# Pooled attention outputs spread and added by TensorE in the prologue, with a new order for prologue and block 0

## What is computed

```python
# q, k, v: (4, 8, 576, 64)
q_d, k_d, v_d = (x.reshape(B, H, 144, 4, D).mean(axis=3) for x in (q, k, v))
out_up = np.repeat(softmax_attention(q_d, k_d, v_d), 4, axis=2)
mask = np.abs(pos[:, None] - pos[None, :]) < 4
out_local = softmax(where(mask, scale * q @ k.T, -1e9)) @ v
x = (out_up + out_local).transpose(0, 2, 1, 3).reshape(2304, 512)
h = x @ w_in                      # (2304, 2048)
out = (h * tanh(softplus(h))) @ w_out
```

## Time and profile before

| what | us |
|---|---|
| median of 3 runs | 493.91 |
| lowest and highest of them | 490.74, 494.74 |
| the profiled execution | 491.38 |
| its span, first to last instruction | 489.6 |
| mean granted TensorE clock | 0.996 |

### The profile page before, as it was taken

The page is one execution under the profiler, slowest core; times in us unless marked ns, Lnnn a source line. Parts: engine busy times, 40 slices in busy tenths (PEclk is TensorE's granted clock), DMA queues, the critical chain, the costliest instruction groups (busy, mean ns, idle before and its releaser), DMA issues.

```text
span 489.6 us, 10818 instructions
## 1 busy us (share of the span) xinstructions
PE 476.7 (97%) x4364; PEld 427.5 (87%) x4364; DVE 238.4 (49%) x495; ACT 201.5 (41%) x434; POOL 112.9 (23%) x188
## 2 busy tenths in 40 slices
PE   7789999999999999999999999999999999999997
PEld 6678988889898989889898989898998998999995
DVE  4867897553663553544535525435355343222220
ACT  3688285644642533524514525234345151201111
POOL 4899524213303303123112022022021010000000
PEclk8999999999999999999999999999999999999999
DMA  7993093222232130430310301101211000100001
GB/s 244 323 385 114 11 313 111 80 88 97 77 109 59 52 109 23 153 109 1 109 39 20 121 14 45 58 1 57 76 47 57 23 0 2 66 0 1 0 1 64
DMA packets 23729, 39.89 MB, mean 81 GB/s; under 512 B 2688, under 2 KB 12160, under 8 KB 23680
## 3 DMA queue, kind: packets, MB, share of 16 engines
q1 hardware_dynamic: 23680, 39.21, 25.0%
HBM read 34.48 MB, written 4.72 MB: 80 GB/s over the span
## 4 chain that ended last, share of the span: by engine, by line
PE 88%; DMA 3%; POOL 3%; issue 3%; SPq 2%; DVE 1%; ACT 0%; POOLq 0%; DVEq 0%
PE banks L716 39%; PE banks L731 39%; PE banks L666 2%; PE banks L647 2%; PE banks L586 2%; PE banks L619 2%; DMA v_in<-in_v 1%; PE banks L601 1%; PE banks L629 1%; DMA k_t<-in_k 1%; DMA w_out_raw<-in_w_out 1%; POOL prob L474 1%; SPq L334 1%; POOL q_halves L445 1%; POOL v_pool L468 0%
## 5 line engine op out<-in xcount | busy, mean ns | idle before, releaser
L946 DVE CAST g_high<-banks 128x384 fp32r<-128x384 f32 x96 | 53.4, 556 | 163.1 <-PE banks L731 123.5
L716 PE MATMUL banks<-x_high,w_in_high 128*128 128x384 f32 x384 | 130.8, 341 | 1.2 <-DVE g_low L948 1.2
L716 PE MATMUL banks<-x_high,w_in_low 128*128 128x384 f32 x384 | 129.4, 337 | 0.0
L716 PE MATMUL banks<-x_low,w_in_high 128*128 128x384 f32 x384 | 128.8, 336 | 0.0
L1139 ACT ACTIVATE banks<-banks 128x384 f32<-128x384 f32 x96 | 45.4, 476 | 196.1 <-PE banks L716 195.9
L731 PE MATMUL banks<-w_out_high,g_high 128*128 128x512 f32 x288 | 115.1, 400 | 0.0
L731 PE MATMUL banks<-w_out_high,g_low 128*128 128x512 f32 x288 | 113.4, 394 | 0.0
L731 PE MATMUL banks<-w_out_low,g_high 128*128 128x512 f32 x288 | 113.1, 393 | 0.0
L474 POOL TENSOR_TENSOR prob<-prob,small 128x432 f32<-128x432 f32 x24 | 22.3, 928 | 255.3 <-DVE small L907 255.3
L716 PEld LDWEIGHTS banks<-x_high,w_in_high 128*128 128x128 f32 x384 | 72.1, 188 | 5.6 <-DVE g_low L948 2.4
L716 PEld LDWEIGHTS banks<-x_low,w_in_high 128*128 128x128 f32 x384 | 72.1, 188 | 2.8
(11 more groups left out here) (72 smaller groups left out, 478.2 us busy)
## 6 DMA issues: line engine op xcount, KB each, us to landing
v_win<-in_v_win SPq DMA_DIRECT2D x24, 256.0 KB, 3.5
v_in<-in_v SPq DMA_DIRECT2D x32, 168.0 KB, 4.2
k_t<-in_k SPq DMA_DIRECT2D x16, 290.0 KB, 4.7
q_t<-in_q SPq DMA_DIRECT2D x24, 192.0 KB, 3.7
out<-stage SPq DMA_DIRECT2D x17, 256.0 KB, 2.3
k_win<-in_k_win SPq DMA_DIRECT2D x20, 216.0 KB, 3.7
w_out_raw<-in_w_out SPq DMA_DIRECT2D x16, 256.0 KB, 5.3
w_in_raw<-in_w_in SPq DMA_DIRECT2D x16, 256.0 KB, 8.4
```

Source lines behind the costliest of these rows:

```text
L716: last = nc.tensor.matmul(hidden[:, g % HB, 0:TB], w, x[:, k, cols], start=(k == 0 and i == 0), stop=(k == KT - 1 and i == 2))
L946: nc.vector.tensor_copy(g_high[:, g % GB], x).then_inc(g_rounded, 1)
```

## The change

1. For units 0 to 3 `pooled_outputs`, `upsample` and `combine` are replaced by `first_outputs`. PE reads each probability four times (a broadcast of step 0), so one matmul has 192 columns in place of 96, and writes straight to the token columns of the band's output. A pass of `spread_outputs` has 6 matmuls; a second pass with the two banks swapped adds the other half of the keys. PE waits for its own first pass before the second, and for the second before the window's matmuls, which now add to what stands there. The factor 1/4 moves into `copy_pooled`.
2. `round_x(n)` of these units waits for `out_ready` in place of `combined`.
3. All five lists of the prologue and of block 0 are in a new order; from block 1 on nothing moves but one pair of maxima.
4. `busy_for_turns` and `busy_for_outputs` calls are partly replaced by `busy_for_products`, zeros that wait for the last softmax of the prologue.

```diff
+                def spread_outputs(n, swap):
                     s = work(n)
+                    for step in range(CHUNKS):
+                        for part in range(2):
+                            i = (0, 1, 2)[step] if part == 0 else (1, 2, 0)[step]
+                            h, r = (2 * i + part) // CHUNKS, 1 - part if swap else part
+                            rows, some = slice(WK * part, WK * part + CK), slice(GQ // 2 * r, GQ // 2 * (r + 1))
+                            last = nc.tensor.matmul(
+                                x_out(n)[D * h:D * (h + 1), r].rearrange("p (t g o) -> p t g o", t=GT, o=POOL),
+                                v_pool[rows, 0, n, D * i:D * (i + 1)],
+                                s["prob_pool_t"][rows, i, :, some].rearrange("p t (g o) -> p t g o", o=1).broadcast_to(
+                                    [CK, GT, GQ // 2, POOL]),
+                                start=not swap and step != 1, stop=False)
+                    last.then_inc(out_spread, 1)
+                def first_outputs(n):
                     pe.wait_ge(prob_copied, 2 * n + 2)
                     if 1 <= n < AHEAD - 1:
                         pe.wait_ge(x_split, n)
+                    pe.wait_ge(v_pooled, n + 1)
+                    spread_outputs(n, False)
+                    pe.wait_ge(out_spread, 2 * n + 1)
+                    spread_outputs(n, True)
+                    pe.wait_ge(out_spread, 2 * n + 2)
+                    window_outputs(n)
...
-                                        start=True, stop=True)
+                                        start=n >= AHEAD, stop=n >= AHEAD or tp == TP - 1 and c == 1)
...
                 def combine(n):
-                    dve.wait_ge(up_ready, n + 1)
-                    nc.vector.scalar_tensor_tensor(up[:, n % 2], out_pool(n)[:, 1], 1.0 / POOL, up[:, n % 2], ALU.mult,
-                                                   ALU.add).then_inc(up_added, 1)
+                    dve.wait_ge(up_ready, n - AHEAD + 1)
+                    nc.vector.tensor_tensor(up[:, n % 2], out_pool(n)[:, 1], up[:, n % 2], ALU.add).then_inc(up_added, 1)
...
                 def round_x(n):
-                    act.wait_ge(combined, n + 1)
+                    if n < AHEAD:
+                        act.wait_ge(out_ready, n + 1)
+                    else:
+                        act.wait_ge(combined, n - AHEAD + 1)
```

More of the change, by code:

```diff
@@ L363, in _ @@
                 load_q(0)
+                load_q(2)
+                load_const()
                 load_v(0)
-                load_const()
                 load_k(0)
+                load_v_win(0)
                 load_w_out(0)
-                load_q(2)
                 load_q(1)
-                load_v_win(0)
                 load_k(1)
+                load_q(4)
                 load_w_in(0)
-                load_q(4)
                 load_v(1)
                 load_k(2)
-                load_w_in(2)
                 load_k(3)
                 load_w_in(1)
+                load_w_out(1)
+                load_w_in(2)
                 load_q(3)
-                load_w_out(1)
+                load_v(2)
                 load_v(3)
-                load_k_win(4)
[L383 to L394, removed]
+                load_v_win(1)
+                load_v_win(3)
+                load_w_in(5)
+                load_w_in(3)
+                load_v_win(2)
+                load_v_win(4)
+                load_w_in(4)
+                load_v(4)
+                load_masks()
+                load_k(4)
+                load_w_out(2)
+                load_k_win(4)
                 for f in range(6, FT):
@@ L514, in _ @@
                 low_in(4)
+                pool_v(4)
                 low_in(5)
@@ L696, in busy_for_outputs, with busy_for_products @@
                     keep_busy(BUSY, out_bank(n)[:, 0, 0:P])
+                def busy_for_products():
+                    pe.wait_ge(shifted, AHEAD)
+                    pe.wait_ge(exp_pool, AHEAD)
+                    keep_busy(BUSY, hidden[:, 0, 0:P])
                 def first_product(j, f, tiles=range(KT)):
@@ L743, in _ @@
                 band_scores(1)
-                pooled_scores(1)
                 keep_busy(BUSY)
                 keep_busy(BUSY)
+                pooled_scores(1)
+                turn_pooled(0)
                 turn_band(0)
                 band_scores(2)
+                first_outputs(0)
                 pooled_scores(2)
-                keep_busy(BUSY)
-                turn_pooled(0)
-                keep_busy(BUSY)
-                turn_band(1)
-                outputs(0)
                 turn_pooled(1)
                 band_scores(3)
+                turn_band(1)
+                busy_for_outputs(1)
                 pooled_scores(3)
+                first_outputs(1)
+                busy_for_turns(2)
                 turn_band(2)
                 turn_pooled(2)
-                busy_for_outputs(1)
-                outputs(1)
-                busy_for_turns(3)
-                busy_for_turns(3)
-                band_scores(4)
-                busy_for_turns(3)
+                busy_for_products()
+                busy_for_products()
+                first_outputs(2)
                 turn_pooled(3)
-                outputs(2)
                 turn_band(3)
-                pooled_scores(4)
-                outputs(3)
+                busy_for_products()
+                busy_for_products()
+                first_outputs(3)
                 first_product(0, 0, range(KT - 1))
```

206 lines of the change are left out of this document (101 added, 105 removed).

## The result

| what | before | changed |
|---|---|---|
| median of 19 executions, us | 493.06 | 496.02 |
| the profiled execution, us | 491.38 | 499.04 |
| its span, us | 489.6 | 497.2 |
| mean granted TensorE clock in it | 0.996 | 0.990 |
| start of the first product in it, us | 32.6 | 40.0 |

The ratio is 1.0054, with an interval of 1.0029 to 1.0078: about 2.6 us slower, inside the forecast's range (494.0, 489.5 to 498.5) and in its class of "within 1%". One of the 19 executions of the changed kernel, at 565.5 us, was slow for a reason of its own (without it the median is 495.5), and the ratio here and all ratios and medians of the experiments leave out such executions. The two profiled executions stand 7.7 us apart, the medians 2.4 to 3.0, so part of what they show is not the change but which execution was profiled; the experiments sort that out.

A forecast was written before the change was run, and what follows sets the result against it. The prologue was taken as a dependence chain through five strict queues, then PE's own time. Profiled 491.4 + 2.0 - 0.8 = 492.6; on the mean, 492.7 + 1.2, rounded to 494.0 us, range 489.5 to 498.5.

The forecast's parts named there:

- +2.0 for the product's start: Prologue: the first product was to start at 34.5 us, 2.0 us later than in the kernel before.
- -0.8: Block 0: PE's 0.5 us at a pooled transpose and 0.3 us of late weight loads were to go.
- wrong if the first product starts ... after 36.5: Sign of a failed forecast: first product before 32.5 or after 36.5 us, or new block 0 PE waits over 0.5.
- the walk: Prologue: durations followed through the changed engine lists, plus 0.6 us for gaps, put the first product at 34.5 us.
- SP: ... nothing: SP's load list: the new wait for `out_ready` was to cost nothing, with 2 MB still in the queue.
- The spread: Units 0 to 3 on PE: 2.5 us a unit against 1.0 before, with 1.55 us saved behind it.
- rival D: Passes on PE: by the page's latency formula, 0.35 us shorter each, -2.1 us in all, 491.9; chance 0.10.
- In the old kernel unit 3's summing lay under the first 18 matmuls, and the new passes stand ahead of them.: Start of the first product: why the spread, even for x at +1.5 and -1.55 us, was not even there.
- Rival A: Prologue: clock at half rate, 1.6 us a unit for units 0, 2 and 3, 4.8 in all, 498.8; chance 0.15.
- Unit 4's keys: SP's loads: these keys were to come at about 30 us, ahead of two low parts of x, hidden.
- Rival B: SP's loads: unit 4's keys land after 33 us; landing at 35 gives +2, 496; chance 0.05.
- rival C: Prologue: ACT and DVE queues overlap better, outputs end at 31.0 us, -1.5 and -0.8, 490.4; chance 0.20.

The follow-up runs named there:

- e12: The change unaltered, measured again on the chip of the last four runs: 495.95 us, ratio 1.0021 to before.
- e1: The changed kernel with one load moved, unit 4's queries going behind unit 3's in SP's list: 492.98 us, ratio 0.9969 to before.
- e7: The changed kernel with unit 4's queries moved behind unit 3's and unit 3 alone summed the old way: 490.91 us, ratio 0.9949 to before.
- e11: e7 without one of the two `busy_for_products` (zeros only) ahead of unit 3's outputs: 491.10 us, ratio 0.9939 to before.
- e3: The changed kernel's spread on PE with all five lists in the order of before: 495.52 us, ratio 1.0032 to before.
- e4: The changed kernel's new lists with the old summing on ACT and DVE: 495.13 us, ratio 1.0030 to before.
- e10: The changed kernel with before's whole load list, the other four lists new: 497.60 us, ratio 1.0074 to before.
- e5: The kernel before with one load moved, unit 4's queries going behind unit 3's: 493.28 us, ratio 0.9966 to before.
- e6: Old summing on ACT and DVE in the new lists, with unit 4's queries moved behind unit 3's: 494.09 us, ratio 0.9992 to before.
- e2: The changed kernel with six more multiplications of zeros on PE ahead of unit 2's band scores: 495.38 us, ratio 1.0012 to before.
- e9: e1 without the zeros PE multiplies after unit 1's band transposes (six calls): 496.43 us, ratio 1.0039 to before.

## Why the prediction was right, and where it was not

- **The time.** 494.0 was forecast, 495.5 to 496.0 measured; sign, class and range are right. The sum behind it is not, so this was in part luck. The sum was for the profiled execution, 492.6, and that came at 499.04. Its two terms were +2.0 for the product's start and -0.8 behind it; measured were +7.4 (40.0 against 32.6; +5.2 in e12) and +0.2. By the forecast's own sign ("wrong if the first product starts ... after 36.5") the walk is wrong for the change as built, in both of its profiles. The range held because it was 9 us wide, drawn for a fall of the clock, and because most executions lose less than the one that was profiled. With the loads in time the terms come nearer: +0.7 and -0.1 in e1, and +1.0 by the medians at equal clock, where the sum said +1.2.
- **The step that failed: "SP: ... nothing".** The walk followed SP's list by kilobytes and looked at one new wait, that for `out_ready`. The wait that `load_q(4)` has had all along, for unit 0's scores, moved ahead of a weight slice, and was not considered. Measured: 4.5 us of waiting in it against 3.0 before, DMA at 242 and 146 GB/s for four microseconds, unit 2's keys at 17.6, PE idle for 1.73. e1 against the change gives its price: 2.5 to 3.0 us by medians, by ratios (1.0054, and 1.0021 in e12, to 0.9969) 2.6 to 4.2. Of this 1.7 to 2.2 us are there at equal clock; the rest is that the change has the lower clock more often.
- **The spread.** Forecast 0.9 a pass and 2.5 a unit. Measured in e1, unit 3: 30.72 to 33.26, 2.5 us; passes 0.93. Of the record of 192 columns I said 0.33 us, worked out from streaming and a tail; the change's records, min/median/max:

```profile
L641 PE MATMUL banks<-prob_pool_t,v_pool x96: 320/324/579, 19.1 to 38.9; 48*64 48x192 f32 x96
```

  The Trainium skill's formula ("TensorE: Matmul & The Clock Gate", section "Single matmul latency") gives 246 ns at this width, and its rival D falls with it.
- **The walk.** With its loads in time (e1) it holds to within a microsecond or so: outputs of unit 0 at 15.3 (forecast 16.1), band maxima of unit 2 at 18.49 ("near 19"), outputs of unit 2 at 26.4 (27.4), of unit 3 at 30.7 (31.4), first product at 33.3 (33.9 before the added 0.6). In the change it does not: unit 0's spread came at 19.1, 3.0 us after the forecast, unit 2's band maxima at 24.1, 5 us after, and the first product at 40.0, 5.5 us after.
- **"In the old kernel unit 3's summing lay under the first 18 matmuls, and the new passes stand ahead of them."** e7 and e11 bear this out in kind: 2 us by the medians, and a kernel faster than both. In the traces unit 3's outputs are 0.9 us shorter on PE; the other 1.0 lies behind the product's start, and 0.7 of it is a wait in block 1 that e1 has and e7 has not (see Block 0).
- **The clock.** Rival A's mechanism came, at 0.15: half clock, from 18 to 28 us, behind the hole, which the walk did not have. It reached into the window of 26 to 34 that I had named, where the mean granted clock was 0.88, just under my bound of 0.9 (1.00 in e12). Unit 0's outputs took 4.1 us in it against 2.4 in e1, so the 1.6 us that I had put on a unit was right, but it met one unit's outputs and not three. Its price in the times is smaller than my 4.8: the two groups of the change's executions lie 2.7 us apart (and 1.5 in e12), and 11 of 30 are in the lower one. Before is there more often, which I could not see from one profile at 0.996.
- **Unit 4's keys** were to come at about 30, hidden. In e1 they came about 28.9. DVE idled 3.1 us for them, but that was not on the chain, which ran over PE. Rival B did not come, and rival C (31.0) neither; its time of 490.4 is near that of e7 and e11, by another way.
- **Block 0.** That the stretch from the first to the third first product stays as long was right (5.65 us in the change, 5.66 before), PE's wait in it fell from 1.2 to 0.4 us, and the waits of the pooled transposes for POOL are gone. But -0.8 is to be seen only where nothing takes it back. PE's waits for g_low in the change have a second member, 1.1 us at about 132 us, in block 1. Its chain there:

```profile
124.73 4.98 DMA out<-stage
...
132.30 0.57 DVE g_low L978
```

  ACT's copy of an output tile waits until the store of an earlier one has left its buffer, and Mish stands behind it. In e1 the wait is 0.7 us, in e7 and e11 there is none, and the time from the first product to the end is 457.0 before, 457.2 in the change, 456.9 in e1, 455.9 in e7 and e11 (488.8 - 32.9). So up to 1.1 us were gained where the store did not collide, and nothing where it did. How much of it the new order of block 0 gave is not shown: e3, with the old lists, is at 456.2, and so is e4 with the new ones. Why the stores fall otherwise in e7 was not tried.

## What to carry to other kernels

A load that waits for a buffer holds every load behind it, so when a load list is reordered, follow each entry's wait (which buffer, when free) and not its bytes alone. A load list and the orders of the engines belong together: the old loads under the new orders were the slowest version of all (e10). When summing work moves onto the engine that bounds the kernel, keep the last unit's off it if the sums of that unit were already hidden. And take several executions' clocks before you trust one profile: here the two profiled executions stood 7.7 us apart and the medians 2.4 to 3.0.

## What the runs showed of the hardware

- TensorE's clock in the prologue differs from execution to execution of one kernel. Half stretches stood at 8 to 12 us in the profiles of before and e1, at 24 to 30 in e5, at 18 to 28 in the change. The group of executions with the lower mean clock is 1.4 to 3.6 us slower than the other (in e4 the two are equal), and its share runs from 1 of 12 (e1, e3) to 12 of 12 (e6) over kernels that differ in little but the work ahead of the first product.
- Behind a hole of 1.73 us in PE's work, with 0.29 busy of 2 us from 16 to 18, the clock stood at 0.91 in that stretch and at 0.50 in the next; in e12 it fell behind a hole of 1.51 us. In e2 it stayed at 1.00 behind a hole of 1.53 us, with 0.47 busy of 2. So the length of the hole alone does not decide.
- The granted clock of a row is not always that of the work in it. In e7 the row from 8 to 10 us says 1.00:

```profile
8.00:10.00 2.00, 2.00 (x43) 1.42 (x43) 0.54 (x1) 0.62 (x1) 0.92 (x3) 1.00 1.02 383
```

  yet the first scores stand in its chain as

```profile
8.58 0.90 PE banks L588 x32
```

  which is what the same 32 records take in the change at 18.44, at a granted 0.50; at full clock, at 15.00 in e1, they take 0.53. The change itself is such a case, and so are e3 and e9. The change's row from 8 to 10 us says 1.00 as well, and its chain has

```profile
8.40 0.90 PE banks L587 x32
...
12.19 0.90 PE banks L587 x32
```

  Near the start of the program the length of known work tells the clock better than the record does, and the mean clock of an execution misses such a stretch.
- PE waiting for its own last matmul costs its weight loads more than its matmuls: in e1 PEld idles 1.8 us in the 4 waits between the passes, 0.45 us each, and as much again ahead of the window's matmuls, while PE is busy 0.50 of the 0.60 us around the first of them (16.0 to 16.6).
